# Turning q, k and the heads' outputs over 64 rows at a time in a fused attention and mixer kernel

## What is computed

```python
q_rot, k_rot = (rotate(q), rotate(k))
scores = scale * np.matmul(q_rot, k_rot.transpose(0, 1, 3, 2))
scores = scores - np.max(scores, axis=-1, keepdims=True)
attn = np.exp(scores)
attn = attn / (np.sum(attn, axis=-1, keepdims=True) + 1e-09)
attn_out = np.matmul(attn, v)
...
x = attn_out.transpose(0, 2, 1, 3).reshape(B, S, H * D)
h = np.maximum(x.transpose(0, 2, 1) @ w_tok1, 0.0) @ w_tok2
u = x + h.transpose(0, 2, 1)
h2 = np.maximum(u @ w_ch1, 0.0) @ w_ch2
out = u + h2
```

## Time and profile before

| | |
|---|---|
| median of 3 runs | 639.66 us (639.15 to 640.34) |
| the profiled execution | 639.26 us |
| its span, first to last instruction | 637.4 us |
| time around the span | 1.9 us |
| PE busy | 621.5 us, 98% |
| DVE busy | 509.9 us, 80% |
| ACT busy | 465.2 us, 73% |
| POOL busy | 341.4 us, 54% |

### The profile page before, as it was taken

How to read it: one execution, slowest core, us unless ns; L and a number is a source line. 1 busy time by engine, 2 the same in 40 slices (tenths; PEclk the granted TensorE clock), 3 DMA queues, 4 the chain that set the end, 5 groups by cost and what they waited for, 6 DMA issues and landing times.

```text
span 637.4 us, 13799 instructions
## 1 busy us (share of the span) xinstructions
PE 621.5 (98%) x4724; PEld 604.5 (95%) x4724; DVE 509.9 (80%) x881; ACT 465.2 (73%) x1018; POOL 341.4 (54%) x316
## 2 busy tenths in 40 slices
PE   4899999999999999999999999999999999999997
PEld 3799999999999999999999999999999999999997
DVE  7899999999999999977385985569935499553895
ACT  5888999988888999976383655776556765567753
POOL 4999999998888887551900002860017800068200
PEclk9999999999999999999999999999999999999999
DMA  4667766676668765406002331000320003100002
GB/s 130 177 152 205 199 161 169 170 188 172 168 180 212 206 172 127 110 20 217 20 1 64 136 99 60 1 2 2 84 75 0 0 0 82 48 27 2 0 3 74
DMA packets 59594, 62.32 MB, mean 98 GB/s; under 512 B 16592, under 2 KB 43856, under 8 KB 59536
## 3 DMA queue, kind: packets, MB, share of 16 engines
q1 hardware_dynamic: 59232, 61.50, 35.4%
q10 hardware_dynamic: 304, 0.07, 0.0%
HBM read 30.77 MB, written 9.44 MB: 63 GB/s over the span
## 4 chain that ended last, share of the span: by engine, by line
PE 95%; DVE 1%; POOL 1%; ACT 1%; issue 0%
PE slot L624 12%; PE rest L657 12%; PE rest L634 9%; PE slot L1359 8%; PE slot L1361 8%; PE slot L1360 8%; PE rest L1359 6%; PE rest L1361 6%; PE rest L1360 6%; PE rest L383 3%; PE rest L585 3%; PE rest L644 2%; PE slot L1391 2%; PE rest L1391 2%; PE rest L224 1%; PE rest L221 1%
## 5 line engine op out<-in xcount | busy, mean ns | idle before, releaser
L1350 POOL TENSOR_TENSOR w_ch_part<-w_ch_sums,w_ch_part 128x512 fp32r<-128x512 f32 x21 | 31.0, 1476 | 173.3 <-ACT w_ch_part L1603 173.3
L997 DVE TENSOR_REDUCE neg_max<-slot 128x1 f32<-128x576 f32 x142 | 106.7, 752 | 6.3 <-PE slot L624 2.0
L1667 ACT ACTIVATE pieces<-h 128x288 fp32r<-128x288 f32 x168 | 73.8, 444 | 49.8 <-PE slot L1361 24.5
L1005 DVE TENSOR_TENSOR pt_lo<-rest,pt_hi 128x512 fp32r<-128x512 f32 x144 | 96.0, 677 | 1.8 <-ACT pt_hi L854 1.3
L657 PE MATMUL rest<-pt_hi,v 128*128 128x256 f32 (+1 forms) x320 | 89.3, 303 | 0.0
L854 ACT ACTIVATE pt_hi<-rest 128x512 fp32r<-128x512 f32 x144 | 84.1, 596 | 5.1 <-PE rest L634 4.2
L1758 DVE TENSOR_TENSOR pieces<-h,pieces 128x288 fp32r<-128x288 f32 x168 | 74.4, 453 | 9.3 <-ACT pieces L1667 8.8
L657 PE MATMUL rest<-pt_lo,v 128*128 128x256 f32 (+1 forms) x256 | 69.7, 295 | 0.0
L847 ACT ACTIVATE prob_a<-slot,neg_max 128x576 f32<-128x576 f32 x78 | 57.9, 743 | 9.8 <-DVE neg_max L997 9.6
L624 PE MATMUL slot<-key,q_hi 128*128 128x288 f32 x252 | 63.5, 333 | 1.5 <-ACT prob_a L847 0.5
L657 PEld LDWEIGHTS rest<-pt_hi,v 128*128 128x128 f32 x320 | 60.3, 188 | 0.2
(11 more groups left out here) (268 smaller groups left out, 2109.3 us busy)
## 6 DMA issues: line engine op xcount, KB each, us to landing
key<-t_hi_k SPq DMA_DIRECT2D x31, 144.0 KB, 2.3
key<-t_lo_k SPq DMA_DIRECT2D x31, 144.0 KB, 2.4
raw_qk<-in_q_dram SPq DMA_DIRECT2D x16, 256.0 KB, 2.6
raw_v<-in_v_dram SPq DMA_DIRECT2D x16, 256.0 KB, 3.1
x_scratch<-x_pair SPq DMA_DIRECT2D x16, 256.0 KB, 2.2
stage_or_x<-x_scratch SPq DMA_DIRECT2D x16, 256.0 KB, 4.1
q_hi<-t_hi_q SPq DMA_DIRECT2D x31, 128.0 KB, 2.4
q_cross<-t_hi_q SPq DMA_DIRECT2D x31, 128.0 KB, 2.4
```

What stands on the lines that cost most here:

```text
L997: dve.tensor_reduce(neg_max[p % 2][:, i:i + 1], slot[g if 2 <= g < 4 else g % 2][:, :, 0:HALF], AX.XY, ALU.max, negate=True).then_inc(maxe ...
L1005: dve.tensor_tensor(pt_lo[:, :, cols], rest[:, bank, :].rearrange("p (j n) -> p j n", j=G), f32(pt_hi[:, 0:G, cols]), ALU.subtract).then_i ...
L1667: act.activation(pieces[:, ring(m), 0, :], source[WEIGHTS[n]][:, ft, :], ACT.Copy).then_inc(piece_hi, 1)
```

## The change

q and k (from pair 1 on) and the heads' outputs are turned over in two instructions a tile, where there was one: rows 0 to 63 of the data with a 64x64 identity, and rows 64 to 127 with another, each a matmul of 64 rows and 64 columns moving. For q and k the results of the two halves go to two banks (`turned_halves`), and ACT and DVE read and write through access patterns that put them together. For the outputs the two halves go to the same columns of a bank, and the second adds to the first: first A's top and B's low halves by turns (A to bank 1, B to bank 2), later A's low and B's top halves. So the sum of v's two parts is made in PSUM. DVE's two sums are gone; DVE multiplies straight from PSUM by the inverse, which POOL did from `o_sum`.

```diff
-    O_BANKS, K_BANKS, Q_BANKS = 1, 2, 2
+    O_BANKS, K_BANKS, Q_BANKS = (1, 2), 2, 2
...
-    def turn_o(pe, h, bank):
-
-        for n, t in enumerate(range(*O_TILES[h])):
-            mm = pe.transpose(columns(bank, W)[:, n * P:(n + 1) * P], ot[:, t * P:(t + 1) * P], ident[:])
-        mm.then_inc(o_ready[h], 1)
...
+    top, low = slice(0, D), slice(D, P)
+
+    def half_turn(pe, to, x, rows, start=True, stop=True):
+
+        return pe.matmul(to, x[rows], ident[rows, rows], start=start, stop=stop, is_transpose=True, skip_group_check=True)
+
+    def o_half(pe, banks, h, n, rows, start, stop):
+        t = O_TILES[h][0] + n
+        return half_turn(pe, rest[:, banks["AB".index(h)], n * D:(n + 1) * D], ot[:, t * P:(t + 1) * P], rows, start, stop)
+
+    def turn_o_first(pe, banks):
+
+        for n in range(G):
+            o_half(pe, banks, "A", n, top, n == 0, False)
+            o_half(pe, banks, "B", n, low, n == 0, False)
+        o_half(pe, banks, "B", G, low, False, False).then_inc(o_half_done, 1)
+
+    def turn_o_second(pe, banks, p):
+
+        pe.wait_ge(o_half_done, p + 1)
+        for n in range(G):
+            mm = o_half(pe, banks, "A", n, low, False, True)
+            o_half(pe, banks, "B", n, top, False, True)
+        mm.then_inc(o_ready["A"], 1)
+        o_half(pe, banks, "B", G, top, False, True).then_inc(o_ready["B"], 1)
+
+    def normalise(dve, p, h, bank):
+
+        a, (t0, t1) = "AB".index(h), O_TILES[h]
+        dve.wait_ge(o_ready[h], p + 1)
+        dve.wait_ge(inv_done, p + 1)
+        if h == "B" and p > 0:
+            dve.wait_ge(x_stored, p * STORED)
+        dve.tensor_tensor(x_pair[:, 1 - a:NG, a, :], columns(bank, (t1 - t0) * D).rearrange("p (t d) -> p t d", t=t1 - t0),
+                          inverse[p % 2][:, t0:t1].unsqueeze(2).broadcast_to([P, t1 - t0, D]), ALU.mult).then_inc(x_made[h], 1)
+
+    def turned_halves(bank):
+
+        return rest[:, bank:bank + 2, 0:NG * D].rearrange("p r (t n) -> p r t n", t=NG)
...
-            normalise(p - 2, "B")
-            normalise(p - 2, "A")
...
-                to = first_q(t * P, (t + 1) * P) if n == "q" and p == 0 else columns(bank, W)[:, t * P:(t + 1) * P]
-                mm = pe.transpose(to, rot[n][:, t].rearrange("p h d -> p (h d)"), ident[:])
+                x = rot[n][:, t].rearrange("p h d -> p (h d)")
+                if p > 0:
+                    for r, rows in enumerate((top, low)):
+                        mm = half_turn(pe, turned_halves(bank)[:, r, t], x, rows)
+                    continue
...
             after_ot(p - 2, "B1")
-            transpose_o(p - 2, "B")
+            transpose_o(p - 2)
             after_lo(p - 1, 3)
             turn(p - 1, 5, 3)
             score(p, 1)
-            after_sum(p - 2, "B")
-            transpose_o(p - 2, "A")
+            transpose_o_rest(p - 2)
             score(p, 2)
             after_lo(p - 1, 4)
             values(p - 1, "A0", 2, 1)
+            after_sum(p - 2, "B")
             after_sum(p - 2, "A")
             turn_tails(p - 1, 1, 1)
...
-        turn_o(pe, "B", 2)
-        turn_o(pe, "A", 0)
+        turn_o_first(pe, (0, 2))
+        turn_o_second(pe, (0, 2), N - 1)
...
-            act.activation(t_hi[n][p % 2][:], columns(bank, WIDE[n]), ACT.Copy,
+            to, turned_x = ((t_hi[n][0][:, 0:S], columns(bank, S)) if p == 0 else
+                            (by_halves(t_hi[n][p % 2][:]), turned_halves(bank)))
+            act.activation(to, turned_x, ACT.Copy,
...
-                ins = dve.scalar_tensor_tensor(out=t_lo[n][p % 2][:], in0=columns(bank, WIDE[n]), scalar=SCALE,
-                                               in1=f32(t_hi[n][p % 2][:]), op0=ALU.mult, op1=ALU.subtract)
+                for r in range(2):
+                    ins = dve.scalar_tensor_tensor(out=by_halves(t_lo[n][p % 2][:])[:, r], in0=turned_halves(bank)[:, r], scalar=SCALE,
+                                                   in1=by_halves(f32(t_hi[n][p % 2][:]))[:, r], op0=ALU.mult, op1=ALU.subtract)
...
-            sum_o(p - 2, "B")
             turned_lo(p - 1, 4, 0)
             maximum(p, 1)
-            sum_o(p - 2, "A")
             turned_lo(p - 1, 5, 3)
+            make_x(p - 2, "B")
+            make_x(p - 2, "A")
             maximum(p, 2)
```

More of the change, by code:

```diff
@@ L258, in attention @@
     O_TILES = {"A": (0, G), "B": (G, TILES)}
[L259 to L263, removed]
+    zeros = sb(ctx, "zeros", [P, NG, D])
+    t_hi = {n: [sb(ctx, f"t_hi_{n}{i}", [P, W], F32R) for i in range(2)] for n in "qk"}
+    t_lo = {n: [sb(ctx, f"t_lo_{n}{i}", [P, W], F32R) for i in range(2)] for n in "qk"}
     key = [sb(ctx, f"key{a}", [P, S], F32R) for a in range(2)]
@@ L301, in attention @@
     pv_ready, ot_done = ({f: sem(f"{what}_{f}") for f in PARTS} for what in ("pv_ready", "ot_done"))
-    o_ready, o_summed = ({h: sem(f"{what}_{h}") for h in "AB"} for what in ("o_ready", "o_summed"))
-    x_done = sem("x_done")
+    o_half_done = sem("o_half_done")
+    o_ready, x_made = ({h: sem(f"{what}_{h}") for h in "AB"} for what in ("o_ready", "x_made"))
     guard_done, inv_done = sem("guard_done"), sem("inv_done")
@@ L452, in store @@
                 return
-            sp.wait_ge(x_done, 2 * p + 2)
+            for h in "AB":
+                sp.wait_ge(x_made[h], p + 1)
             sp.dma_start(x_scratch[p][0:MAIN, :].rearrange("(p t) c -> p t c", t=G),
@@ L583, in transposes @@
             for t in range(NG):
-                to = first_q(t * P, (t + 1) * P) if n == "q" and p == 0 else columns(bank, W)[:, t * P:(t + 1) * P]
-                mm = pe.transpose(to, rot[n][:, t].rearrange("p h d -> p (h d)"), ident[:])
-                if n == "q" and p == 0 and t == EARLY - 1:
+                x = rot[n][:, t].rearrange("p h d -> p (h d)")
[3 more added lines that the diff above has]
+                    continue
+                to = first_q(t * P, (t + 1) * P) if n == "q" else columns(bank, W)[:, t * P:(t + 1) * P]
+                mm = pe.transpose(to, x, ident[:])
+                if n == "q" and t == EARLY - 1:
                     mm.then_inc(first_turned, 1)
@@ L659, in values, with transpose_o, transpose_o_rest @@
             mm.then_inc(pv_ready[f], 1)
-        def transpose_o(p, h):
+        def transpose_o(p):
             if no(p):
                 return
-            if h == "A":
-                pe.wait_ge(ot_done["A0"], p + 1)
-                pe.wait_ge(ot_done["A1"], p + 1)
-            else:
-                pe.wait_ge(ot_done["A1"], p + 1)
-                pe.wait_ge(ot_done["B0"], p + 1)
-                pe.wait_ge(ot_done["B1"], p + 1)
-            turn_o(pe, h, O_BANKS)
+            for f in PARTS:
+                pe.wait_ge(ot_done[f], p + 1)
+            turn_o_first(pe, O_BANKS)
+        def transpose_o_rest(p):
+            if not no(p):
+                turn_o_second(pe, O_BANKS, p)
         def after_lo(p, i):
@@ L691, in after_sum @@
             if not no(p):
-                pe.wait_ge(o_summed[h], p + 1)
+                pe.wait_ge(x_made[h], p + 1)
         pe.wait_ge(consts, 4)
@@ L1125, in last_sums @@
         for h, bank in (("B", 2), ("A", 0)):
-            dve.wait_ge(o_ready[h], N)
-            dve.wait_ge(x_done, 2 * N - 2)
-            dve.tensor_reduce(o_sum[h][:], o_halves(h, bank), AX.X, ALU.add).then_inc(o_summed[h], 1)
+            normalise(dve, N - 1, h, bank)
     def last_store(sp):
-        sp.wait_ge(x_done, 2 * N)
+        for h in "AB":
+            sp.wait_ge(x_made[h], N)
         sp.dma_start(x_scratch[N - 1][0:MAIN, :].rearrange("(p t) c -> p t c", t=G),
```

54 lines of the change are left out of this document (19 added, 35 removed).

## The result

The changed kernel takes **646.15 us** (median of 4, 645.52 to 646.71) against 640.00 (639.15 to 640.93) on the same chip: ratio 1.0095, 95% interval 1.0078 to 1.0113. I had forecast 630.0, 623 to 645. It became slower by 6.15 us, outside the range and on the other side.

What follows compares the result with a forecast made beforehand. PE was taken to bound the kernel, DVE close behind. PE alone would gain 0.7 us a pair, DVE allowed 0.6: 8.4 us over 14 pairs, 9.5 with the parts outside, giving 630 us, range 623 to 645.

Steps and rivals of the forecast that it cites:

- What bounds the kernel: Attention pairs: PE, busy for the whole 17.20 us, sets the pace, with DVE only 0.6 us behind.
- (a): PE's turns of q, k and outputs: two halves run side by side in 57 ns, gaining 0.91 us a pair.
- my sign of being right: In the changed profile, turns of 64 columns on PE about 28 ns from start to start.
- (b): Before A's turning, PE's wait for B's sum on DVE goes: gain 0.17 us a pair.
- (c): PE's new wait for `x_made` ahead of the tails costs about 0.4 us a pair, bounds 0 and 0.6.
- (d): DVE gets 0.38 us a pair shorter, needs 16.2, and allows a pair of 16.6 us, 0.6 less.
- (e): ACT's `t_hi_k` grows 0.06 us and POOL loses 1.3 us a pair of multiplications: no effect on time.
- the sum: Whole kernel: the smaller gain, DVE's 0.6 us a pair over 14 pairs, 8.4 us; with the parts outside, 9.5.
- PE empties itself at each change of rows: Rival: PE drains between 128 and 64 rows, at most 164 ns each, 8 times a pair; 643 us, chance 0.18.
- serial halves: Rival: PE's half turns run one after the other, 57 ns each; 638.5 us, chance 0.13.
- the sequencer: Rival: PE's sequencer can't keep up, two halves taking 124 ns instead of 109; 641.5 us, chance 0.07.
- DVE holds more: Rival: DVE can't use its 0.6 us, gain 0.3 a pair, 634 us; chance 0.62 shared with forecast and half drain.

Runs made afterwards that it cites:

- b_one_whole: The kernel before the change, with one extra whole turn of 128 rows ahead of k's turning, 14 times: 639.74 us, ratio 1.0003.
- a_make_first: The changed kernel with DVE's two multiplications behind the low parts of tiles 4 and 5 after the loop, ahead of tile 5's inside it: 641.79 us.
- d_block: The changed kernel with q and k whole, and one long 64-row block a pair for the outputs and probability tiles 4 and 5: 652.37 us, ratio 1.0204.

## Why the prediction was wrong

**What bounds the kernel: half right.** PE does set the pace, but "busy for the whole 17.20 us" was read as "no hole", and there were two large ones, the sum's 0.18 that I had seen and 0.22 ahead of the tails' scores, where PE stands for ACT (and two of 0.03 to 0.05, 53 ns behind DVE's low parts of q and k). b_one_whole shows it: 0.109 us of PE a pair more for 0.04 us in all.

**(a) The halves' price: right,** 0.92 for 0.91 us a pair, without their edges. If the ninth half of a block is counted as a whole step, as in (a), it is 0.87: a step takes 60 ns where I had 57. 28 ns a half was my sign of being right, and it was there (30).

**(b) The sum wait: gone, but replaced.** The place that waited 0.18 us for DVE now waits 0.16 for the edge.

**(c) The new wait: real, over-priced.** 0.4 us a pair forecast, 0.14 measured at the place, some 2.3 us in the loop by a_make_first. PE came later than I had it, which I put down to the edges. I didn't look behind the loop, where the same order of DVE's work cost another 1.7.

**(d), (e) DVE, ACT and POOL: sizes right, effect overlooked.** I had looked at the sum of DVE's work and not at who waits for its parts: PE waits for the low part of q, which became two instructions, 0.085 us a pair more than before. The multiplications take 482 and 415 ns (forecast 485 and 418), DVE's pair 16.24 us (16.2). These are its groups after, against the earlier trace rows:

```profile
L411 DVE TENSOR_TENSOR x_pair<-rest,inverse 128x320 f32<-128x320 f32 x16 | 7.7, 482 | 6.2 <-PE rest L382 6.2
L411 DVE TENSOR_TENSOR x_pair<-rest,inverse 128x256 f32<-128x256 f32 x16 | 6.6, 415 | 0.0
```

**The step that failed** is that the sum puts a change between 128 and 64 rows at nothing. It stood only in the first rival, *PE empties itself at each change of rows*: I gave that 0.18 and had its price bounded at 164 ns an edge, 1.3 us a pair; measured is 0.15 to 0.197 an edge, 1.37 a pair, more than the 0.92 + 0.17 gained. I let it go on a weak argument: that a change in loaded columns, 128 to 64, costs nothing. That said nothing of rows, as I noted myself, and in the changed kernel the same two facts stand side by side: the tails' 64 columns are free and the 64 rows are not. The rule that I cited from the Trainium skill (TensorEngine Tiling (Array Packing), Key Properties), that a change of the tiling mode drains the engine, agrees with this trace: 39 waits at line 382, 0.16 us in the mean, for nothing else that it shows. The rival's 643 falls 3 us short of the 646: it had taken the new wait as covered (2.3) and had nothing behind the loop (1.7) and nothing for DVE's low part of q (1.2), and the hole ahead of the tails' scores gave 0.17 a pair back (2.4). So its nearness is in part luck. The rivals of serial halves and of the sequencer are out: 302 ns for ten. That DVE holds more is not what decided: its waits, 0.14 and 0.085 us a pair, are small beside the edges' 1.37.

What stays open: whether a long block would pay if ACT's queue didn't stand behind it (d_block changed both, so it doesn't say), and why d_block's block gained less than its halves and edges add up to.

## What to carry to other kernels

Price a change of shape by its edges as well as its work: here an edge between 128 and 64 rows costs 0.15 to 0.20 us, a half turn saves some 24 ns (20 of them save 0.49 us), so by this estimate a block with its two edges, 0.31 to 0.37 us, breaks even at about 14 halves, and these held 9 and 10. No run shows a block that pays: the one of 34 halves did not. Before calling an engine full, look at starts and not at busy time: where records are longer than the pitch, holes of up to the difference don't show. Where a hole has no name in the profile, look for an instruction of another engine that ends the same time ahead of it in every round of the loop. And when work moves between engines in a kernel with an order written by hand, check the code behind the loop, whose order is another one.

## What the runs showed of the hardware

- Two turns on different row halves of the array start 3 to 6 ns apart; ten halves take 302 ns from first to last start, five whole turns 435.
- In the serial order, five upper halves and then five lower ones, ten take 418 ns; by the long record of the third start the lower ones start ahead of their place in the program.
- A change of rows shows in the load: it starts some 70 ns before the record ahead ends, instead of 2 ns behind that one's start, and isn't hidden (first record 273 ns instead of 223, or 328 instead of 273).
- An f32 product of 64 columns is issued as two instructions 112 ns apart, where a turn of 128 columns is one of 109.
- Hand-overs to PE are constant: its load starts 53 ns after the end of the low part that it waits for on DVE, and 112 to 114 ns after the sum's read that ends an exponential on ACT.
